# An attention stage unrolled and reordered, with its reciprocals spread by transfers through DRAM

## What is computed

```python
def _attn_ref(q, k, v, tau):
    scale = 1.0 / np.sqrt(q.shape[-1])
    scores = scale * np.matmul(q, k.transpose(0, 1, 3, 2))
    thresh = np.max(scores, axis=-1, keepdims=True) - tau
    scores = np.where(scores >= thresh, scores, -1000000000.0)
    scores = scores - np.max(scores, axis=-1, keepdims=True)
    attn = np.exp(scores)
    attn = attn / (np.sum(attn, axis=-1, keepdims=True) + 1e-09)
    return np.matmul(attn, v)

# then, with x = attn_out as [4, 576, 512]:
#   u = x + (x^T U V)^T ;  x = u + relu(u w_ch1) w_ch2
#   gate = sigmoid(causal convolution of x, 5 taps) ;  out = (gate * (x w_val)) w_out
```

## Time and profile before

| | |
|---|---|
| time, median of 3 runs | 856.79 us (856.43 to 857.83) |
| the profiled execution's own time | 857.68 us |
| its span | 855.8 us |
| busy: PE, PEld | 832.7, 770.6 us |
| busy: DVE, ACT, POOL | 441.1, 398.5, 410.5 us |
| granted TensorE clock, mean | 0.996 of full |
| attention stage | from the start to about 313 us |

### The profile page before, as it was taken

The page is one execution under the profiler, slowest core; times in us unless marked ns, Lnnn a source line. Parts: engine busy times, 40 slices in busy tenths (PEclk is TensorE's granted clock), DMA queues, the critical chain, the costliest instruction groups (busy, mean ns, idle before and its releaser), DMA issues. The chain is left out here.

```text
span 855.8 us, 19088 instructions
## 1 busy us (share of the span) xinstructions
PE 832.7 (97%) x6864; PEld 770.6 (90%) x6864; DVE 441.1 (52%) x981; ACT 398.5 (47%) x1013; POOL 410.5 (48%) x306
## 2 busy tenths in 40 slices
PE   5999999999999989999999999999999999999998
PEld 4888888888888869989999999999999999989987
DVE  6899999999999855312231122411123223384231
ACT  5999999999999833221121211112111112243231
POOL 5998777677770120064082560834707338091000
PEclk9999999999999999999999999999999999999999
DMA  7544334433331012200000000000000102032221
GB/s 178 125 111 110 81 95 117 114 81 81 91 97 53 13 38 87 62 2 28 1 2 28 1 29 1 0 28 0 28 1 1 53 13 90 12 113 93 90 78 62
DMA packets 27726, 48.89 MB, mean 57 GB/s; under 512 B 5344, under 2 KB 14112, under 8 KB 27680
## 3 DMA queue, kind: packets, MB, share of 16 engines
q1 hardware_dynamic: 24944, 43.54, 18.6%
q10 hardware_dynamic: 2736, 4.72, 1.5%
HBM read 38.81 MB, written 8.85 MB: 56 GB/s over the span
## 5 line engine op out<-in xcount | busy, mean ns | idle before, releaser
L883 DVE SCALAR_TENSOR_TENSOR h_lo<-psum,h_hi 128x288 fp32r<-128x288 f32 x128 | 58.6, 458 | 287.8 <-ACT h_hi L816 287.8
L816 ACT ACTIVATE h_hi<-psum 128x288 fp32r<-128x288 f32 x128 | 52.7, 412 | 255.2 <-PE psum L753 255.2
L751 PE MATMUL psum<-u_split,w_hi 128*128 128x288 f32 x512 | 158.0, 309 | 3.1 <-PEq L166 3.1
L753 PE MATMUL psum<-u_split,w_lo 128*128 128x288 f32 x512 | 152.2, 297 | 0.0
L752 PE MATMUL psum<-u_split,w_hi 128*128 128x288 f32 x512 | 151.9, 297 | 0.0
L516 DVE SCALAR_TENSOR_TENSOR probs<-psum,thresh,exp_scores 128x576 f32<-128x576 f32 (+1 forms) x160 | 129.0, 807 | 8.4 <-ACT exp_scores L396 2.4
L507 DVE TENSOR_REDUCE neg_max<-psum 128x1 f32<-128x576 f32 (+1 forms) x160 | 120.5, 753 | 16.6 <-PE psum L285 13.4
L396 ACT ACTIVATE exp_scores<-psum,neg_max 128x576 f32<-128x576 f32 (+1 forms) x160 | 117.7, 735 | 0.0
L284 PE MATMUL psum<-qk_split 128*128 128x288 f32 (+1 forms) x320 | 105.5, 344 | 10.4 <-DVE qk_split L495 9.4
L751 PEld LDWEIGHTS psum<-u_split,w_hi 128*128 128x128 f32 x512 | 97.0, 189 | 6.9 <-issue 6.9
L752 PEld LDWEIGHTS psum<-u_split,w_hi 128*128 128x128 f32 x512 | 96.9, 189 | 3.6 <-issue 3.6
(11 more groups left out here) (119 smaller groups left out, 1816.0 us busy)
## 6 DMA issues: line engine op xcount, KB each, us to landing
qk_raw<-in_qk SPq DMA_DIRECT2D x60, 288.0 KB, 4.3
out<-o_sb ACTq DMA_DIRECT2D x18, 256.0 KB, 2.0
w_stage<-in_w SPq DMA_DIRECT2D x16, 256.0 KB, 2.7
v_main<-in_v SPq DMA_DIRECT2D x16, 256.0 KB, 2.7
conv<-in_w SPq DMA_DIRECT2D x16, 256.0 KB, 2.6
conv_dram<-conv SPq DMA_DIRECT2D x7, 576.0 KB, 2.8
gates<-conv_dram SPq DMA_DIRECT2D x7, 576.0 KB, 3.6
probs<-in_qk SPq DMA_DIRECT2D x4, 288.0 KB, 4.8
```

The source lines that it names most:

```text
L751: nc.tensor.matmul(out, w1_hi[:, cols], u_hi[:, half, d], start=(d == 0), stop=False)
L753: mm = nc.tensor.matmul(out, w1_lo[:, cols], u_hi[:, half, d], start=False, stop=(d == DB - 1))
```

## The change

The loops over steps and pairs are written out, for all engines, so that all counts are constants (wait, step_loop and pair_loop go). Three things move beside that.

- Reciprocals. ScalarE's spreading copy, the second transpose of transpose_tails and half of the tail copy go. SP writes the two columns of row_inv to a DRAM tensor, inv_dram, waits until they have landed, and reads them back with each row repeated for 64 partitions, into inv_rows, which has three slots. normalise multiplies by inv_rows and comes one step later.
- Banks. Head 0's main transposes stay in bank 6, where the tails follow them; head 1's go to bank 7, before the value products of the same step.
- Order. Head 1's transposes move one step later, and most of the order within a step changes. SP's loads are cut into single ones and set between the transfers of the reciprocals.

```diff
-    T_BANK, O_BANK = 6, 7
+    T_BANKS, TAIL_BANK, O_BANK = [6, 7], 6, 7
...
+            def spread_inverse(m):
+                rows, c = Q_ROWS[m % QB], 2 * (m % QB)
+                sp.wait_ge(inv_done, m + 1)
+                until(sp, inv_in[m % 3], 16 * (m // 3))
+                sp.dma_start(inv_dram[m % 3].rearrange("a q -> q a")[0:rows], row_inv[0:rows, c:c + 2],
+                             allow_slow_non_contiguous=True).then_inc(row_out, 16)
+                sp.wait_ge(row_out, 16 * (m + 1))
+
+                until(sp, o_evac, m - 2)
+                sp.dma_start(inv_rows[:, m % 3, 0:rows],
+                             inv_dram[m % 3, :, 0:rows].unsqueeze(1).broadcast_to([2, D, rows])
+                             ).then_inc(inv_in[m % 3], 16)
...
-            pair_loop(sp, load, 0)
...
+            for p in range(3):
+                load_v(p)
+            for m in range(STEPS):
+                p, j = divmod(m, QB)
+                spread_inverse(m)
+                if m in (1, 2):
+                    load_qk(2, m - 1, 0)
+                    load_qk(2, m - 1, 1)
+                if j >= 3 and p + 3 < PAIRS:
+                    load_qk(p + 3, 0, j - 3)
+                if j < 2 and 3 <= p + 2 < PAIRS:
+                    load_qk(p + 2, 1, j)
+                if j == 2 and 3 <= p + 2 < PAIRS:
+                    load_v(p + 2)
+                if j == 2 and p > 0:
+                    load_w1(p)
+                if p == PAIRS - 2 and j == 4:
+                    load_mixing()
...
+            def transpose_main(m, a):
                 n, rows = 2 * m + a, Q_ROWS[m % QB]
-                wait(pe, probs_done, n + 1, 2 * BODY, t)
-
-                wait(pe, t_evac, n, 2 * BODY, t)
+                pe.wait_ge(probs_done, n + 1)
+
+                if a:
+                    until(pe, o_evac, m)
+                else:
+                    until(pe, tail_evac, m)
...
-                wait(pe, o_evac, m, BODY, t)
-                wait(pe, inv_spread, m + 1, BODY, t)
-                nc.tensor.transpose(psum[:, O_BANK, P:P + rows], probs[0:rows, m % 3, KM * P:KM * P + P],
-                                    ident[0:rows, 0:rows])
-                mm = nc.tensor.transpose(psum[:, O_BANK, 2 * P:2 * P + rows], inv_cols[0:rows, m % 3],
-                                         ident[0:rows, 0:rows])
-                mm.then_inc(tail_ready, 1)
+                pe.wait_ge(probs_done, 2 * m + 2)
+
+                pe.wait_ge(t_evac, 2 * m + 1)
+                nc.tensor.transpose(psum[:, TAIL_BANK, 0:rows], probs[0:rows, m % 3, KM * P:KM * P + P],
+                                    ident[0:rows, 0:rows]).then_inc(tail_ready, 1)
...
-            def spread_inverse(m, t):
-                rows, c = Q_ROWS[m % QB], 2 * (m % QB)
-                wait(act, inv_done, m + 1, BODY, t)
-
-                wait(act, tail_ready, m - 2, BODY, t)
-                nc.scalar.copy(inv_cols[0:rows, m % 3].rearrange("p (a d) -> p a d", a=2),
-                               row_inv[0:rows, c:c + 2].unsqueeze(2).broadcast_to([rows, 2, D])
-                               ).then_inc(inv_spread, 1)
...
+            for i in range(STEPS + 3):
+                if 0 < i <= STEPS:
+                    threshold(2 * i - 2)
+                    exponent(2 * i - 2)
                 if 0 <= i - 2 < STEPS:
-                    spread_inverse(i - 2, t)
-                if 0 <= i - 3 < STEPS:
-                    evac_tails(i - 3, t)
+                    guard_sums(i - 2)
+                if i >= 3:
+                    evac_main(i - 3, 0)
+                if i % QB == 1 and i > QB:
+                    w1_high(i // QB - 1)
                 if 0 < i <= STEPS:
...
+            def normalise(m):
                 rows, q0 = Q_ROWS[m % QB], PAD + Q_START[m % QB]
-                wait(dve, o_ready, m + 1, BODY, t)
...
+                dve.wait_ge(o_ready, m + 1)
+                dve.wait_ge(inv_in[m % 3], 16 * (m // 3 + 1))
+                nc.vector.tensor_tensor(x_t[:, m // QB, q0:q0 + rows], psum[:, O_BANK, 0:rows],
+                                        inv_rows[:, m % 3, 0:rows], ALU.mult).then_inc(o_evac, 1)
...
+            for i in range(STEPS + 4):
+                if 0 < i <= STEPS:
+                    weights(2 * i - 2)
+                if i >= 4:
+                    normalise(i - 4)
+                if 0 <= i - 2 < STEPS:
+                    reciprocal_sums(i - 2)
                 if i < STEPS:
-                    maximum(2 * i, t)
+                    maximum(2 * i)
                 if 0 < i <= STEPS:
-                    weights(2 * i - 1, t)
...
                 if i < STEPS:
...
+                    maximum(2 * i + 1)
```

More of the change, by code:

```diff
@@ L52, in until @@
         engine.wait_ge(sem, value)
[L55 to L80, removed]
 def overlay(nc, ctx, *layouts):
@@ L99, in stages, with attention @@
     return [flat[:, 0:DM], flat[:, DM + P // 2:2 * DM + P // 2]], flat[:, DM:DM + S]
-def attention(nc, ctx, qk, v, tau, w1, u4, v4, w2, conv_w, psum, x_t, w1_hi, w1_lo, ident, mixing, u_split, free,
+def attention(nc, ctx, inv_dram, qk, v, tau, w1, u4, v4, w2, conv_w, psum, x_t, w1_hi, w1_lo, ident, mixing, u_split, free,
               conv, cw, heads):
@@ L109, in attention @@
     v_main = sb("v_main", [P, 3, KM, P])
-    stage, v_tail, inv_cols, probs, e_sb = free
-    pt = sb("probs_t", [P, 3, 2 * KM + 2, P])
+    stage, v_tail, probs, e_sb = free
+    inv_rows = sb("inv_rows", [P, 3, P])
+    pt = sb("probs_t", [P, 3, 2 * KM + 1, P])
     one = sb("one", [P, 1])
@@ L168, in _, with load_qk, load_v @@
         def _(sp):
[L169 to L178, removed]
+            def load_qk(p, a, h):
+                sp.wait_ge(split_ready, 2 * p + a - 3)
+                sp.dma_start(raw[D * h:D * h + D, a], qk[p * 2 + a]).then_inc(qk_in[a], 16)
+            def load_v(p):
+                until(sp, o_ready, QB * (p - 2))
                 sp.dma_start(v_main[:, p % 3],
-                             v[pair, 0:KM * P].rearrange("(k p) d -> p k d", p=P)).then_inc(v_in[p % 3], 16)
+                             v[p, 0:KM * P].rearrange("(k p) d -> p k d", p=P)).then_inc(v_in[p % 3], 16)
                 for a in range(2):
@@ L252, in work, with w1_low @@
                 if p > 1:
[L253 to L258, removed]
+                    until(pool, split_ready, 2 * p)
+                    w1_low(p - 2)
+            def w1_low(c):
+                until(pool, w1_hi_done, c + 1)
+                cols = slice(c * DM, (c + 1) * DM)
                 nc.gpsimd.tensor_tensor(w1_lo[:, cols], stage[:], w1_hi[:, cols].bitcast(F32),
                                         ALU.subtract).then_inc(w1_lo_done, 1)
-            pair_loop(pool, work, 1)
+            for p in range(1, PAIRS):
+                work(p)
             for c in (PAIRS - 2, PAIRS - 1):
                 pool.wait_ge(w1_lo_done, c)
-                w1_low(c, None)
+                w1_low(c)
             for d in (0, 1):
@@ L1155, in build @@
             with ExitStack() as stage:
-                attention(nc, stage, qk, v, tau, w1, u4, v4, w2, conv_w, psum, x_t, w1_hi, w1_lo, ident, mixing,
-                          u_split, (w1_stage, v_tail, inv_cols, probs, e_sb), conv, cw, heads)
+                attention(nc, stage, inv_dram, qk, v, tau, w1, u4, v4, w2, conv_w, psum, x_t, w1_hi, w1_lo, ident, mixing,
+                          u_split, (w1_stage, v_tail, probs, e_sb), conv, cw, heads)
             with ExitStack() as stage:
```

225 lines of the change are left out of this document (98 added, 127 removed).

## The result

The kernel after takes 1346.26 us (median of 4 runs, 1342.38 to 1350.36), the kernel before 857.2 beside it: ratio 1.571, interval 1.567 to 1.575. The forecast was 918 us, 872 to 965. The sign was right; of a loss of 489 us it saw 61.

What follows compares the result with a forecast made beforehand. In attention TensorE's weight loads, VectorE and ScalarE were nearly full, none alone the limit; a ring through two engines ended last in long steps. SP's transfers added 58 us: 857.7 + 58 + 3 - 0.9 = 918 us, range 872 to 965.

Steps and rivals of the forecast that it cites:

- The write: 2.6 us: SP's write of row_inv to DRAM: 0.85 + 1.4 + 0.35 = 2.6 us to land, low end 1.3.
- 0.35 us is the way back: End of a DMA transfer: 0.35 us from its last packets to its landing, read from the last store.
- Small packets cost an engine 82 ns: Rival for the broadcast on two engines: 5.2 us, a step of 7.7, over 1,000 us in all; chance 0.05.
- The broadcast on two engines: Read back into inv_rows: two engines carry 128 packets, 1.73 us, landing after 3.1; 918 us, chance 0.62.
- The order in the rings: DMA packets queue behind earlier ones: in a step with a qk_raw, 4.17 us from one broadcast's issue to the next.
- The fifth step: The one step in five issuing v_main, two v_tail and w_stage: SP itself is the path, 5.6 us.
- high end (26.4, 973 us): Broadcast packets at 44 ns: steps of 5.2 and 5.6, a pair of 26.4, 973 us in all.
- The low end's "about 4.9": Packets at 24.5 ns and the short write: steps of 4.0, the fifth about 4.9, a pair of 20.9, 899 us.
- Steps without loads are hidden (3.3 us): Later attention steps, without loads on SP: a broadcast can follow another after 3.3 us, which is hidden.
- SP's pace sets the stage: Attention: normalise waits for the transfers, next maxima and second head's transposes for it; a pair takes 22.3 us against 17.95.
- unrolling at nothing: Loops written out for all engines: costed at nothing on both sides, since no step is longer where the loop turns over.
- The engines gain 0 to 19 us: Computing engines in attention: long steps can fall to 3.33 us, 1.26 us a pair, 19 over 15 pairs, or gain nothing.

Runs made afterwards that it cites:

- the writes apart: Kernel after with each write's 4-byte elements 64 B apart in their own DRAM tensor, the broadcast reading a compact tensor of ones: 990.08 us, step 5.20.
- without transfers: Kernel after without the transfers of the reciprocals, values multiplied by ones held in SBUF: 842.24 us, step 3.39.
- late_read: Kernel after with the broadcast of a step issued after the write of the next one: 1284.25 us, step 8.97.

## Why the prediction was wrong

- **The write: 2.6 us.** This step failed. It measured 8.2 (8.3 alone). The packets were even quicker than forecast: alone, all 272 were through 1.2 us after the issue, where 0.85 + 1.4 = 2.25 was said. What was wrong is "0.35 us is the way back": alone it was 7 us. The 0.35 was read from a store in whole rows, and the 4-byte price from tau, which is written to SBUF. No row showed small elements written to DRAM, and here they lie next to each other. The write got a low end (1.3) and a middle, and no high end: nothing in the trace bounded it above, and the range should have said so. In the sum: 9.77 - 5.20 = 4.57 us a step, times 80, 366 us (356 measured).
- **"Small packets cost an engine 82 ns"**, the one rival over 1,000 us (0.05), came nearest in size, by a cause that isn't there. The packets occupy engines hardly at all; none is moving in the last 5 us.
- **The broadcast on two engines: right.** In the 1.48 us from 771.80 of the profile after, with only its packets:

```profile
DMA  1011110101111010111101011110101111010111
...
q1 hardware_dynamic: 125, 0.06, 14.3%
```

  If two engines carry them, 125 packets in 1.48 us are 62 on each, 24 ns apart, as dense as v_main's 24.5; the share, 14.3%, is close to two engines' 12.5%. That it is two shows in the count from 771.40 to 773.50 above: of its 274 small packets 256 are elements and 16 the write's completions, and 2 are left for the broadcast. Alone it landed in 3.24 us (forecast 3.1). The rule of the Trainium skill (DMA: Bandwidth & Descriptors, "Why a DMA increments its semaphore by 16 and not by 1") holds here. But cutting the broadcast over 16 engines made both kernels slower.
- **The order in the rings, 4.17 us a step with a load: too low.** With the writes apart it measured 5.44, from the broadcast's issue at 209.75. The packets of the write are over at 214.18, after 4.43 us (forecast 3.76), and the landing is 1.0 us behind them (forecast 0.35, the same value that failed above). The window from 213.10 to 214.20 of that kernel, behind which no packet follows until 215.18:

```profile
DMA  9949932111312711216000040050000101011010
...
q1 hardware_dynamic: 214, 0.04, 26.7%
```

  The fifth step came as forecast, 5.7 us (median) against 5.6. The four with a load took 4.9 to 5.5, so a pair took 26.8 instead of 22.3. That is what the prediction has as its high end (26.4, 973 us), which its range of 872 to 965 leaves out. So even without the cost of neighbours the time, 990 us, would have lain outside. In totals, 990 is 133 us over the kernel before, where the forecast had 61, and 148 over the 842 without transfers. The low end's "about 4.9" for the fifth step isn't worked out in the prediction: its terms give 2.93 + 1.3 + 0.06 = 4.3, and 891 us instead of 899.
- **Steps without loads are hidden (3.3 us): right for the mechanism.** 3.54 with the writes apart, which is hidden beside the old step but not quite beside the new order's 3.39; in after mostly 8.6 to 9.2, since the write is that long everywhere. This is why the last pairs, too, lost.
- **SP's pace sets the stage; normalise waits for inv_rows: right.** So were the later stages (548 us against 542) and unrolling at nothing (-1.1 us).
- **The engines gain 0 to 19 us**: 14.3 without transfers.

The same page of the Trainium skill says, under "Anatomy of one DMA", that the wait until the written data are confirmed can be "a surprisingly long delay especially when the write target is HBM". The section describes transfers issued by GpSimd, and these are issued by SP, but it would have pointed at the right term. The runs here agree only in part: DRAM as such isn't it, since two rows of 512 B landed in 1.1 us, and 256 separate elements 64 B apart in 1.6.

## What to carry to other kernels

Price a transfer by its landing and take that only from a transfer with the same destination, element size and neighbourhood; where the trace has none, the cost has no upper end, and the range must say so or the transfer be measured alone first. Don't write single elements next to each other into DRAM on a path that something waits for: transpose on TensorE, or lay them 64 B apart if the reader can take them so (no run here reads them back). A wait for one's own write in the queue that also carries the loads makes every landing a term of the step.

## What the hardware showed unexpectedly

- 256 writes of 4 bytes into DRAM: 7.9 to 8.5 us side by side, 4.3 to 4.6 with starts 8 B apart, 1.7 to 2.4 at 16 B, 1.7 to 2.6 at 32 B, 1.5 to 1.8 from 64 B on (once 3.0). Pairs of 8 B side by side, 128 packets: 4.3 to 4.5.
- Loads issued behind such a write are late: in late_read qk_raw took 11.1 us instead of 4.6. The DMA engines look busy meanwhile: their packets fill 59% of the stage and move 43 GB/s, where those of after fill 20% at 39 GB/s and those with the writes apart 32% at 75. So there a busy DMA engine is not one that moves much.
- TensorE, idle for 351 of the stage's 784 us, was granted 0.70 of its clock over the stage (1.00 before), a mix of its two levels, 2.4 and 1.2 GHz: its transposes took 377 ns on average, and 263 in the kernel without transfers. It didn't cost here, since SP's queue was the path and waited for a reciprocal under 1 us in all.
